# Four 32-column matmuls side by side for the recurrence's outputs and state update

## The reference

```python
for t in range(S):                       # S = 768, per batch and head, D = 40
    m_new = maximum(f_gate + m, i_gate)
    f_stab = exp(f_gate + m - m_new)
    i_stab = exp(i_gate - m_new)
    C = f_stab * C + i_stab * outer(v, k)        # 40 x 40 state
    n = f_stab * n + i_stab * k                  # 40 state
    h = C @ q
    y[t] = sigmoid(o_gate) * h / maximum(abs(n . q), 1)
x = moe(x):   (sigmoid(x @ w_gate) * (x @ w_val)) @ w_out          # 320 -> 1536 -> 320
x = moe2(x):  rms norm, then (silu(xn @ w_gate) * (xn @ w_val)) @ w_out
```

## Time and profile before

| | before |
|---|---|
| time, median of 3 runs | 450.05 us (450.0 to 450.38) |
| the profiled execution's own time | 450.07 us |
| its span, first to last instruction | 448.2 us |
| TensorE busy | 444.2 us, 99% of the span |
| VectorE, ScalarE, GpSimd busy | 215.6, 183.7, 87.2 us |
| granted TensorE clock | 1.00 |

### The profile page before, as it was taken

The page is one execution under the profiler, slowest core; times in us unless marked ns, Lnnn a source line. Parts: engine busy times, 40 slices in busy tenths (PEclk is TensorE's granted clock), DMA queues, the critical chain, the costliest instruction groups (busy, mean ns, idle before and its releaser), DMA issues.

```text
span 448.2 us, 10567 instructions
## 1 busy us (share of the span) xinstructions
PE 444.2 (99%) x4494; PEld 405.5 (90%) x4494; DVE 215.6 (48%) x475; ACT 183.7 (41%) x358; POOL 87.2 (19%) x131
## 2 busy tenths in 40 slices
PE   9999999999999999999999999999999999999997
PEld 5899999999999999988889988889988899888897
DVE  6876927854556456424432227560055630256510
ACT  7885377534753473214543154331033320223310
POOL 3567710112010200004656181000000000000000
PEclk9999999999999999999999999999999999999999
DMA  8975600221122114000433010000000000000000
GB/s 235 308 257 144 163 3 3 82 82 38 48 80 69 37 31 153 8 2 20 142 106 117 17 44 1 1 1 29 31 2 0 1 16 29 16 2 1 1 29 29
DMA packets 10430, 26.69 MB, mean 60 GB/s; under 512 B 1504, under 2 KB 4608, under 8 KB 10384
## 3 DMA queue, kind: packets, MB, share of 16 engines
q1 hardware_dynamic: 10128, 25.96, 18.9%
q10 hardware_dynamic: 256, 0.07, 0.1%
HBM read 23.97 MB, written 1.97 MB: 58 GB/s over the span
## 4 chain that ended last, share of the span: by engine, by line
PE 99%; ACT 0%; issue 0%; DVE 0%
PE bank L1218 37%; PE bank L1169 21%; PE bank L1237 10%; PE bank L1238 9%; PE bank L1239 9%; PE bank L1076 3%; PE bank L1107 3%; PE bank L1010 2%; PE bank L1249 1%; PE bank L1095 1%; PE bank L1046 1%; PE bank L1116 1%; PE bank L1264 0%; PE bank L1256 0%; PE bank L1272 0%; PE bank L1060 0%
## 5 line engine op out<-in xcount | busy, mean ns | idle before, releaser
L1218 PE MATMUL bank<-x_hi,wgv_hi 64*128 64x512 f32 x576 | 105.8, 388 | 0.0
L689 ACT ACTIVATE sg<-bank 128x256 f32<-128x256 f32 (+1 forms) x96 | 47.1, 492 | 131.2 <-PE bank L1218 82.5
L1218 PE MATMUL bank<-x_lo,wgv_hi 64*128 64x512 f32 x480 | 93.8, 386 | 0.0
L960 DVE TENSOR_TENSOR bank<-sg,bank 128x256 f32<-128x256 f32 (+1 forms) x96 | 53.8, 560 | 58.0 <-ACT sg L689 56.5
L1169 PE MATMUL bank<-x_hi,wgv_hi 128*128 128x256 f32 x288 | 80.4, 290 | 0.0
L1169 PE MATMUL bank<-x_lo,wgv_hi 128*128 128x256 f32 x288 | 77.7, 282 | 0.0
L1237 PE MATMUL bank<-wo_hi,h_hi 128*128 128x320 f32 x240 | 75.4, 314 | 0.0
L1218 PE MATMUL bank<-x_hi,wgv_lo 64*128 64x512 f32 x384 | 75.1, 386 | 0.0
L1239 PE MATMUL bank<-wo_hi,h_lo 128*128 128x320 f32 x240 | 74.1, 309 | 0.0
L1238 PE MATMUL bank<-wo_lo,h_hi 128*128 128x320 f32 x240 | 74.1, 309 | 0.0
L1218 PEld LDWEIGHTS bank<-x_hi,wgv_hi 64*128 64x128 f32 x576 | 54.4, 184 | 11.5 <-issue 0.7
(11 more groups left out here) (143 smaller groups left out, 538.7 us busy)
## 6 DMA issues: line engine op xcount, KB each, us to landing
step<-in_qk_t SPq DMA_DIRECT2D x24, 192.0 KB, 3.8
step<-in_vok SPq DMA_DIRECT2D x12, 324.0 KB, 3.2
step<-in_w_gv SPq DMA_DIRECT2D x6, 576.0 KB, 3.6
raw_x<-in_w_gv SPq DMA_DIRECT2D x4, 576.0 KB, 7.9
raw_p<-in_w_gv SPq DMA_DIRECT2D x4, 576.0 KB, 5.8
step<-in_vok SPq DMA_DIRECT2D x10, 160.0 KB, 5.8
raw_p<-in_w_o SPq DMA_DIRECT2D x3, 480.0 KB, 3.3
y<-y_tok SPq DMA_DIRECT2D x9, 160.0 KB, 1.8
```

What stands on the lines that cost most here:

```text
L689: act.activation(sg_view(n), g_view(n), ACT.Sigmoid).then_inc(sg_done, 1)
L960: dve.tensor_tensor(v_view(n), sg_view(n), v_view(n), ALU.mult).then_inc(hf_done, 1)
L1218: mm = pe.matmul(ps(n), w, x, start=own and (s, p) == (0, 0), stop=last and not own)
```

## The change

In N, each head's 128 columns are taken as four quarters of 32 instead of two halves of 64. In K, each head's 40 columns are taken as 32 and 8, so that they lie on two 32-column parts; the two groups of heads together use all four. The values that are computed, the tiles and the waits are the same, and no other engine's program is touched.

```diff
@@ N
-                            for u in range(2):
-                                us = slice(HALF * u, HALF * u + HALF)
+                            for u in range(P // Q):
+                                us = slice(Q * u, Q * u + Q)
                                 mm = pe.matmul(bank[base(n) + 2][us, h * D1:(h + 1) * D1], wexp[b][:, h, us],
                                                va[b][:, h * D1:(h + 1) * D1], start=True, stop=True)
@@ K
-                            mm = pe.matmul(kv_view(n)[HALF * i:HALF * i + D, c * D1:(c + 1) * D1], kn[b][:, h * D:(h + 1) * D],
-                                           vk[b][:, h * D1:(h + 1) * D1], start=True, stop=True)
+
+                            for d0, d1 in ((0, Q), (Q, D)):
+                                mm = pe.matmul(kv_view(n)[HALF * i + d0:HALF * i + d1, c * D1:(c + 1) * D1],
+                                               kn[b][:, h * D + d0:h * D + d1], vk[b][:, h * D1:(h + 1) * D1],
+                                               start=True, stop=True)
```

## The result

| | before | after |
|---|---|---|
| time, median | 450.22 us (450.0 to 450.47, 4 runs) | 459.9 us (459.04 to 460.3, 4 runs) |
| the profiled execution's own time | 450.07 us | 459.04 us |
| its span | 448.2 us | 457.1 us |
| TensorE busy | 444.2 us, 99% | 444.0 us, 97% |

The ratio is 1.0215, with an interval from 1.0203 to 1.0227: slower by 2.1%, where 0.7% faster was forecast, and outside the range of 445.0 to 450.3.

What follows compares the result with a forecast made beforehand. The prediction took TensorE, busy 444.2 of 448.2 us, to bound the kernel. 3.44 us from N in the weave + 0.17 at the start - 0.25 for a wait gave 3.36, rounded 3.4: 446.7 us, range 445.0 to 450.3.

Steps and rivals of the forecast that it cites:

- The step of four: N in the weave: 16 steps a chunk of four records, 37 ns for 58.5; 0.34 us a chunk, 3.44 in ten.
- K: State update: 8 steps of four at 37 ns for 37.5, no gain; new shape avoids a gap of some 0.1 us before N.
- The start: N of chunks 0 and 1: the last eight steps after VectorE's product at 12.38 get shorter, 0.17 us gained.
- VectorE's wait: N of chunks 0 and 1: TensorE waits longer for VectorE's products, its first idle time between 11.5 and 12.4 us.
- The wait at 52 us: First block's last weight piece: TensorE, now early, waits for GpSimd's split; 0.25 us given back.
- The sum: Whole kernel: N's weave gain plus the start's gain less the wait for GpSimd, 3.36 us, rounded 3.4.
- rival 2: N and K: records can't start closer than 14.6 ns; N gains nothing, K loses 1.3 us, 451.4 us; chance 0.11.
- No row shows a longer burst: Argument for rival 2: the densest row, I's at 14.6 ns a record, runs over 32 records only.
- The Trainium skill's overhead of about 60 cycles for each matmul: N and K: 25 ns for each record one after another, N 1.6 us a chunk, K 0.8, some 460 us; rejected.

Runs made afterwards that it cites:

- e8: e5 with N's matmuls of chunks 4 to 11 streaming 21 of their 41 columns, the rest of N's output left out; 447.84 us in one run.
- e1: Kernel before with only K in parts of 32 and 8 columns, N left in halves of 64; 451.38 us, ratio to before 1.0026.
- e2: Kernel before with only N in quarters of 32 columns, K left in one matmul of 40; 453.36 us, ratio to before 1.0070.
- e11: Changed kernel with one 576 KB load of layer 0's weights issued later at the start; 456.84 us in a single run.
- e10: Changed kernel with two 576 KB loads of layer 0's weights issued later at the start; 457.88 us, ratio to before 1.0173.
- e3: Changed kernel with the eight long filler matmuls at the start written as 84 short ones, 152 instructions more; 450.58 us, ratio to before 1.0007.
- e5: Changed kernel with the smaller parts of N and K only from chunk 4 on, earlier chunks as before; 447.72 us, ratio to before 0.9943.
- e7: e5 with the smaller parts from chunk 3 on instead of chunk 4, 96 instructions more; 452.92 us, ratio to before 1.0060.

## Why the prediction was wrong

- **The step of four.** Right in kind: as many steps, four records in each. 37 ns were taken and 40 measured, 0.34 us a chunk against 0.28: 0.6 us in ten chunks. The cause of that difference is open. The working had the stream as the later of the two, 35 ns against 30.5 for the weights; e8, 3 ns a step for half the stream, shows that the stream isn't the limit. That 37 came near 40 rests on the row of K from which it was taken, and in part on luck.
- **K.** Right: 0.31 us for 0.34, and the gap that its new shape avoids is 0.09 to 0.13 us in e1 and e2.
- **The start.** 0.17 us of gain against 4.8 + 0.23 of loss. VectorE's wait came where it was expected, 0.21 us at 12.1 us. The block's was not foreseen, and the lower clock came with it: the wait of 3.15 us had it behind it, those of 1.24 and 0.69 us in e11 and e10 had not.
- **The wait at 52 us.** 0.25 us for GpSimd's split were expected. There is a wait at 54.34, 1.05 us, but a block's: the fetch ended at 54.02 and TensorE went on at 55.54, 1.5 us behind, as everywhere. One row names VectorE's h_lo for it, which had been done by 54.95. The wait for GpSimd doesn't show in e2 and e3 either, where chunk 3's N is short and no block's wait stands there: TensorE has no idle time from 48 to 62 us in their views. That term came out as nothing.
- **The step that failed.** The sum, 3.44 + 0.17 - 0.25 us, has no term for the supply of TensorE's instructions; it was put at nothing. What the runs showed in its place are 9.0 us of "issue" waits at N, nearly all of them for blocks, 1.0 more at 54 us and 1.1 us of slower fillers behind the first. The supply was named only in rival 2, "If TensorE's supply of instructions ends there". There it was priced as a rate, 14.6 ns a record as in the densest row, with 1.3 us as its worst and a chance of 0.11. The objection to it, that four records start at once, was right and beside the point: the supply has no such rate. It comes in blocks of 256 instructions, one ahead, and what counts is how long TensorE takes to use a block up and where in a dense stretch the block ends. "No row shows a longer burst" was the warning. The page's row of q8 and the doubled record counts would have let 224 instructions be compared with 320 and with 256, and the fetch near the start, with 3.2 us of room before, was to be had from the trace.
- **The Trainium skill's overhead of about 60 cycles for each matmul** (TensorEngine Tiling (Array Packing), section Performance Considerations) gave an estimate of some 460 us, close to 459.9, for another reason. Its 25 ns a record don't add up here: N's records start 10 ns apart, and e5 with 512 of N's records in quarters is faster than before. Rejecting that sum was right and the time it gave was no support for it.

## What to carry to other kernels

Cutting a matmul into more, smaller ones is paid in instructions. Before doing it, add up the instructions (two for each record) of the densest stretch and compare with a block of 256: if a block is used up in less than about 3.5 us, TensorE is likely to stop at its end (it did at most such ends here, and not at chunk 10's, whose next fetch had begun early), so look in the trace for "issue" as what it waited for, on whatever line happens to begin the block. Its cost then depends on where the blocks end, so a hundred or so instructions more or less anywhere ahead can move the time by several us (96 cost 5.2 us in e7, 152 gained 9.3 us in e3), and a version that uses the small matmuls only in some places can be faster than all or none. A fetch also stands behind the loads that are queued already, so dense stretches and crowds of loads shouldn't meet.

## What the runs showed of the hardware

- TensorE's records can start 10 ns apart on average, weight loads included, for at least 64 records in a row (0.75 us to the next line in chunk 3), when four 32-column matmuls stand side by side.
- TensorE's instructions come in 16 KB blocks of 256, one ahead; a fetch mostly takes 0.9 to 1.5 us, and its first instruction runs 1.24 us after its end at the earliest.
- A fetch waits for the loads queued before it: block 2's began at 13.69, 12.25 and 11.00 us with none, one and two loads of 576 KB taken away ahead of it, and at 13.39 and 11.53 us in the kernel before.
- Going between parts of 32 and of 64 columns costs TensorE 0.09 to 0.13 us, either way (e1, e2).
- The granted clock read 0.93 and 0.81 in the two stretches around and behind the wait of 3.15 us at the start, and the fillers there started 0.43 us apart and not 0.22, as at the 1.2 GHz level; behind the waits of 1.24 and 0.69 us in e11 and e10 they kept the full rate.
